# One more split step of q and k, and three casts moved from GpSimd to VectorE

## What is computed

```
qn = q / (norm(q, axis=1) + 1e-6);  kn = k / (norm(k, axis=1) + 1e-6)   # q, k, v: 1 x 6016 x 256
a = softmax(kn.T @ qn / tau);  x = v @ a                                # a: 256 x 256
x = mlp1(x)   # h = x @ w_in (256 x 2048); h * sigmoid(1.702 h); @ w_out (2048 x 256)
x = mlp2(x)   # the same shapes, with ELU
```

## Time and profile before

| | |
|---|---|
| median of 3 runs | 1028.44 us (1028.13 to 1028.62) |
| the profiled execution's own time | 1028.24 us |
| its span, first to last instruction | 1026.5 us |
| TensorE busy | 1021.6 us (100%) |
| VectorE, ScalarE busy | 762.3 us, 760.4 us (74% each) |
| GpSimd busy | 37.0 us (4%), all of it in the first 50 us |
| granted TensorE clock | 1.000 over the span |

### The profile page before, as it was taken

The page is one execution under the profiler, slowest core; times in us unless marked ns, Lnnn a source line. Parts: engine busy times, 40 slices in busy tenths (PEclk is TensorE's granted clock), DMA queues, the critical chain, the costliest instruction groups (busy, mean ns, idle before and its releaser), DMA issues.

```text
span 1026.5 us, 14103 instructions
## 1 busy us (share of the span) xinstructions
PE 1021.6 (100%) x4650; PEld 861.5 (84%) x4650; DVE 762.3 (74%) x1247; ACT 760.4 (74%) x1364; POOL 37.0 (4%) x39
## 2 busy tenths in 40 slices
PE   9999999999999999999999999999999999999998
PEld 8988888888888888889998888888888888888997
DVE  6897756565656565655888988887888788788776
ACT  7996665575666566556688888888888788888875
POOL 6800000000000000000000000000000000000000
PEclk9999999999999999999999999999999999999999
DMA  9921012002003002003113002102102000110111
GB/s 360 306 41 42 1 42 42 1 36 47 1 1 80 1 1 60 1 1 124 42 62 99 1 1 62 21 1 62 21 1 62 9 14 24 35 21 1 21 22 36
DMA packets 103434, 46.25 MB, mean 45 GB/s; under 512 B 87170, under 2 KB 94018, under 8 KB 102722
## 3 DMA queue, kind: packets, MB, share of 16 engines
q1 hardware_dynamic: 100816, 44.38, 15.7%
q10 hardware_dynamic: 2546, 0.98, 0.4%
HBM read 33.03 MB, written 12.32 MB: 44 GB/s over the span
## 4 chain that ended last, share of the span: by engine, by line
PE 98%; DMA 1%; POOL 0%; SPq 0%; DVE 0%; issue 0%; ACT 0%; DVEq 0%
PE bank L1241 32%; PE bank L1242 32%; PE bank L1243 32%; PE bank L1251 1%; DMA qk<-in_k_dram 1%; POOL qk_lo L472 0%; PE bank L1356 0%; PE bank L1357 0%; PE bank L1361 0%; SPq L362 0%; PE bank L1334 0%; PE bank L1501 0%; PE bank L1264 0%; DVE blocks L1220 0%; DVE xo L1230 0%
## 5 line engine op out<-in xcount | busy, mean ns | idle before, releaser
L1241 PE MATMUL bank<-g_hi,w_dn_hi 128*128 128x512 f32 (+1 forms) x768 | 296.2, 386 | 0.1
L1242 PE MATMUL bank<-g_lo,w_dn_hi 128*128 128x512 f32 (+1 forms) x768 | 295.8, 385 | 0.0
L1243 PE MATMUL bank<-g_hi,w_dn_lo 128*128 128x512 f32 (+1 forms) x768 | 295.7, 385 | 0.0
L992 DVE TENSOR_TENSOR g_lo<-gated,g_hi 128x512 fp32r<-128x512 f32 (+1 forms) x384 | 259.4, 677 | 47.6 <-ACT g_hi L667 41.7
L1241 PE MATMUL bank<-blk_hi,w_up_hi 128*128 128x512 f32 (+1 forms) x672 | 259.0, 385 | 0.0
L1243 PE MATMUL bank<-blk_hi,w_up_lo 128*128 128x512 f32 (+1 forms) x672 | 258.9, 385 | 0.0
L1242 PE MATMUL bank<-blk_lo,w_up_hi 128*128 128x512 f32 (+1 forms) x672 | 258.8, 385 | 0.0
L667 ACT CAST g_hi<-gated 128x512 fp32r<-128x512 f32 (+1 forms) x289 | 176.3, 610 | 20.5 <-DVE gated L979 20.4
L1241 PEld LDWEIGHTS bank<-g_hi,w_dn_hi 128*128 128x128 f32 x768 | 144.2, 188 | 28.3 <-DVE g_lo L992 1.1
L1243 PEld LDWEIGHTS bank<-g_hi,w_dn_lo 128*128 128x128 f32 x768 | 144.2, 188 | 27.0
L1242 PEld LDWEIGHTS bank<-g_lo,w_dn_hi 128*128 128x128 f32 x768 | 144.2, 188 | 26.6
(11 more groups left out here) (130 smaller groups left out, 777.5 us busy)
## 6 DMA issues: line engine op xcount, KB each, us to landing
x_scratch<-xo SPq DMA_DIRECT2D x10, 512.0 KB, 3.1
raw<-x_scratch SPq DMA_DIRECT2D x5, 1024.0 KB, 5.6
out_dram<-blocks SPq DMA_DIRECT2D x40, 128.0 KB, 2.8
qk<-in_q_dram SPq DMA_DIRECT2D x12, 384.0 KB, 10.4
qk<-in_k_dram SPq DMA_DIRECT2D x12, 384.0 KB, 11.1
stage<-in_moe_w_in_dram SPq DMA_DIRECT2D x8, 512.0 KB, 8.1
stage<-in_moe_w_out_dram SPq DMA_DIRECT2D x8, 512.0 KB, 3.9
blocks<-in_v_dram SPq DMA_DIRECT2D x32, 128.0 KB, 3.3
```

Of the source, the lines that this page charges most:

```text
L992: nc.vector.tensor_tensor(g[1][:, x, 0:w], gated[:, n % 2, 0:w], g[0][:, x, 0:w].bitcast(F32), ALU.subtract).then_inc(c_glo, 1)
L1241: nc.tensor.matmul(out_ps, w_hi, x_hi, start=start, stop=False, skip_group_check=goes_on)
L1242: nc.tensor.matmul(out_ps, w_hi, x_lo, start=False, stop=False, skip_group_check=goes_on)
L1243: return nc.tensor.matmul(out_ps, w_lo, x_hi, start=False, stop=stop, skip_group_check=goes_on)
```

## The change

A third step of the groups is split in group 13: its step 1 was multiplied whole and is now split. The casts of step 1 of groups 12, 13 and 14 are made by VectorE, in front of its additions of groups 11, 12 and 13. GpSimd no longer casts for groups 12 and 14, waits for VectorE's cast (`c_qkhi3`), and makes one subtraction more, that of group 13's step 1.

```diff
-    TWICE = [4, 6, 8, 10, 12, 14]
+    TWICE = [4, 6, 8, 10, 12, 13, 14]
+
+    CAST_BY_VECTOR = [12, 13, 14]
...
+        c_qkhi3 = sem("c_qkhi3")
...
             for i, (n, step) in enumerate(SPLITS):
-                if step:
+                if step and n in CAST_BY_VECTOR:
+                    pool.wait_ge(c_qkhi3, CAST_BY_VECTOR.index(n) + 1)
+                elif step:
                     pool.wait_ge(c_qk[n % RING], qk_count(n))
                     if i >= PARTS:
                         pool.wait_ge(c_score, SPLITS[i - PARTS][0] + 1)
                     nc.gpsimd.tensor_copy(qk_hi[:, i % PARTS, :, :], qk[:, n % RING, :, step, :]).then_inc(c_qkhi2, 1)
-                    pool.wait_ge(c_qkhi2, TWICE.index(n) + 1)
+                    pool.wait_ge(c_qkhi2, [m for m in TWICE if m not in CAST_BY_VECTOR].index(n) + 1)
...
             for n in range(LANES):
+
+                m = n + 1
+                if m in CAST_BY_VECTOR:
+                    i = SPLITS.index((m, 1))
+                    dve.wait_ge(c_qk[m % RING], qk_count(m))
+                    if i >= PARTS:
+                        dve.wait_ge(c_score, SPLITS[i - PARTS][0] + 1)
+                    nc.vector.tensor_copy(qk_hi[:, i % PARTS, :, :], qk[:, m % RING, :, 1, :]).then_inc(c_qkhi3, 1)
                 dve.wait_ge(c_sq, n + 1)
                 dve.wait_ge(c_sum, SUM_ZERO + n)
```

## The result

The changed kernel takes 1031.56 us in the median of 6 runs, against 1028.48 of the kernel before: ratio 1.0033, 95% interval 1.0017 to 1.005. It is slower by 0.3%. The forecast was 1030.0 and no change that can be told; the median lies in the stated range, but beyond the 1030.5 above which the prediction called it slower. And it spreads: its six runs go from 1029.30 to 1033.83 us, where the six of the kernel before lie between 1027.83 and 1028.62.

The account below looks back on a forecast made before the run. TensorE, busy nearly throughout, was taken to bound the kernel. 1028.24 us plus 1.6 us of TensorE lateness gave 1029.8, or 1030.0 against the median of the runs; range 1028.2 to 1031.7 us.

Parts of the forecast that it names:

- What bounds the kernel: TensorE, busy 1021.6 of 1026.5 us: lateness in the first 45 us stays, since the 980 us behind hold no gap.
- TensorE's own gain, 0.14 us: Group 13's second step split on TensorE: 2.30 instead of 2.44 us, 0.14 us off, all the gain there is.
- The cast beside GpSimd: VectorE's three SBUF casts beside busy GpSimd: middle case taken, turns by instruction, each between 0.42 us and a longer wait.
- rival 1: VectorE's casts run beside GpSimd at 0.42 us each: +0.13 us, 1028.4 to 1028.6 us; chance 0.30.
- Rival 2: GpSimd keeps access between instructions, VectorE casts only when GpSimd waits: TensorE +2.85 us, 1031.1 or 1031.3; chance 0.27.
- The turns, step by step: VectorE's casts alternate with GpSimd's subtractions: group 13's addition at 32.47 against 29.70, 2.77 us late, TensorE 1.6 late.
- The path through ScalarE: ScalarE squares group 15 2.54 us late, then casts groups 17 and 18 late, delaying GpSimd's subtractions that TensorE needs.
- the folds: VectorE's last fold ends at 43.14, just ahead of `norms` at 43.24, so TensorE does not wait for it.
- TensorE goes on at 42.5 where it was at 40.92: +1.6 us: TensorE at group 18, after GpSimd's last subtraction ends at 42.41: 1.6 us late, the whole forecast cost.
- rival 3: Something else moves, such as TensorE stalls lowering its clock or group 12 landing late; chance 0.07, of it 0.04 slower.
- The chances: Whole kernel: slower by over 0.2% 0.36, within 0.2% 0.62, faster 0.02; the forecast itself had 0.36.

Follow-up runs that it names:

- psum_cast: The changed kernel with VectorE's three casts made as additions of zeros from PSUM; 1029.52 us, ratio 1.0011.
- split_only: The changed kernel with the third split step kept but all casts made by GpSimd, none by VectorE; 1030.61 us, ratio 1.0021.
- again: The changed kernel without any edit, run for a second profile and more runs; 1032.39 us, ratio 1.004.
- filled: The changed kernel with 3 and 4 small unused products on TensorE ahead of its waits for the low parts of groups 17 and 18; 1030.87 us, ratio 1.0024.
- two_casts: The changed kernel with group 12's cast left on GpSimd, so VectorE casts only for groups 13 and 14; 1029.74 us, ratio 1.0015.
- stall_07: The kernel before with one TensorE wait added ahead of group 18's split step, until VectorE's low part of w_in; 1029.68 us, ratio 1.0015.

## Why the prediction was wrong

- **What bounds the kernel:** right. Each tenth of a microsecond that TensorE is late at 41 us is in the span.
- **TensorE's own gain, 0.14 us:** right, 2.30 against 2.44 us for group 13.
- **The cast beside GpSimd:** right in kind. The two exclude each other by whole instructions, so rival 1 is out. That they take turns the first profile shows: the second cast got in between the subtractions of 27.47 and 28.71, though the latter had its operands. The Trainium skill's rule in "SBUF — State Buffer", section "Who interferes with whom", is the exclusive lock that the prediction cites: the trace agrees with the casts of 1.09 to 1.41 us in place of 0.42. The same section says that a VectorE instruction with at most one SBUF input, outside the two-port forms, does not contend with GpSimd; the 0.68 us of `psum_cast` agree. It also says that a VectorE instruction with two SBUF inputs contends with a GpSimd one that reads SBUF; the 2.01 us of L897 in `split_only` agree.
- **Rival 2 in the late case:** `again` alone could not have told it from the forecast. There each cast ends right ahead of the subtraction that needs it, with two subtractions to a cast, as the prediction had drawn rival 2, and the addition of group 13, at 33.20, is nearer to rival 2's 33.7 than to the forecast's 32.47. Turns give this picture too: GpSimd's next instruction is the one that waits for the cast.
- **The turns, step by step:** the size came out on both sides of mine. I had one path, with VectorE 2.77 us late and TensorE 1.6. There are at least two, set by whether the first cast starts 0.05 us ahead of a subtraction or 0.17 behind it: 1.94 and 0.74 us late (1029.3), or 3.50 and 2.29 (the runs of 1030.7 to 1031.0 at the full clock, as far as `filled` shows). The second is beyond the 3.2 us of VectorE that the prediction named as the point from which TensorE is over 2 us late. The path through ScalarE was right in both: TensorE waits for the low part of group 18, in the late case for that of group 17 too, and the folds do not delay `norms`.
- **The step that failed** is "TensorE goes on at 42.5 where it was at 40.92: +1.6 us", on two counts. I reckoned with one path where there are two, and the later one, which all ten runs of `filled` took by their times, makes TensorE 2.29 us late. And the sum took a wait of TensorE for its own length and no more: there the clock was missing. I had read the 1.00 of the earlier trace rows as given, while behind waits it was 0.50 for some us in a share of the runs; a fall stood only in rival 3, at a chance of 0.04 together with others. It cost 3.07 us in the profile of `again`, more than the 2.29 by which TensorE was late. Seven of the 11 runs of the changed kernel have a clock of 0.998 or less, so it decides the median. Without it, in the late case, the kernel is at 1030.87 (`filled`), still slower by 0.24% and above the 1030.5 that I had drawn as the border. So of the way from the forecast's 1030.0 to the measured 1031.56 and 1032.39, by `filled` about 0.9 us are the turns and the remaining 0.7 and 1.5 the clock.
- **The chances:** 0.36 for slower was too low for both reasons. I had given the forecast's path one case in six above 1030.5, and the late case lies there even at the full clock; and the clock had almost no weight. The upper end of the range, 1031.7, leaves out all seven runs with a fallen clock. That the first median, 1031.56, lies inside is no merit of the sum: it is the mean of a run at the full clock and one at 0.998.

No version that beats the kernel before came out. The split is worth 0.14 us, each way to feed it costs TensorE a longer wait at the end of the stage, and the best one with the split, `psum_cast`, is still 1.1 us behind.

## What to carry to other kernels

Before work is moved to VectorE beside a busy GpSimd, look at its operands: a cast from SBUF to SBUF that takes 0.42 us alone took 1.0 to 1.4 us there when it started behind a GpSimd instruction, and held up GpSimd too, while the nominally slower form with one operand in PSUM took its 0.68. And a wait on a TensorE that had none is priced at its length plus, in a share of the runs, some microseconds of half clock behind it; a median over several runs, or each run's clock, shows that, and one profile may not. Where such a wait could not be avoided, products that compute nothing were cheaper here than the bare wait.

## What the runs showed that I had not expected

Waits of 1.32 and 0.62 us, with 0.6 us of work between them, were followed by half the clock from 43.5 to 50 us; waits of 0.21 and 0.62 us (`two_casts`) by about 3 us of it, to 47.5. A single wait of 0.8 us (`stall_07`) was followed by a lower mean clock in one run of 11, one of 2.2 us in three of 5, and that of 0.61 us in `psum_cast` in none of 11. Whether the clock falls differs from run to run of the same kernel, and what decides it the runs do not show. And the landing of one group of data differs between profiles by 0.6 us (the first cast began at 25.93, 26.09, 26.24, 26.50 and 26.54); in the kernel before it does little harm, to judge by its runs, which lie within 1.1 us: TensorE is four microseconds behind the landings. The changed kernel made it count by letting VectorE's cast wait for it beside GpSimd.
